# The first sort of a scan and two expert layers split in two, its first part beside the scan

## The reference

```
# attention: x, f_logit are (2, 5056, 256)
f = lower_bound + (1 - lower_bound) * sigmoid(f_logit);  i = 1 - f
for t in range(S):  h = f[:, t] * h + i[:, t] * x[:, t];  y[:, t] = h
# layer 0: N = 10112 tokens, D = 256, E = 8 experts, F = 1024
logits = (x/|x|) @ (emb/|emb|).T / tau;  expert_idx = argmax(logits)
out[mask_e] = gate_w * (relu(x[mask_e] @ w1[e]) @ w2[e])     # gate_w: softmax value of the chosen one
# layer 1: the same with logits = x @ w_gate and its own w1, w2
```

## Time and profile before

| | us |
|---|---|
| median of 3 runs | 1384.75 (1382.49 to 1385.55) |
| the profiled execution | 1383.36 |
| its span | 1381.6 |
| PE busy | 1329.6 (96%) |
| DVE busy | 971.5 (70%) |
| ACT busy | 835.2 (60%) |
| POOL busy | 439.2 (32%) |

### The profile page before, as it was taken

How to read it: one execution, slowest core, us unless ns; L and a number is a source line. 1 busy time by engine, 2 the same in 40 slices (tenths; PEclk the granted TensorE clock), 3 DMA queues, 4 the chain that set the end, 5 groups by cost and what they waited for, 6 DMA issues and landing times.

```text
span 1381.6 us, 31343 instructions
## 1 busy us (share of the span) xinstructions
PE 1329.6 (96%) x11005; PEld 1299.6 (94%) x11005; DVE 971.5 (70%) x1468; ACT 835.2 (60%) x1402; POOL 439.2 (32%) x458
## 2 busy tenths in 40 slices
PE   7994799999999999999999999999999999999996
PEld 6993399999999999999999999899999999999996
DVE  5878476666666666669876679777777777777773
ACT  4774166666666666666656566556666666666663
POOL 4663221121221211222111234323444444444431
PEclk9995599999999999999999999999999999999999
DMA  8983686666665656668856668546666666666650
GB/s 256 329 275 104 64 273 193 213 199 194 203 198 200 199 195 214 198 193 154 254 166 192 209 202 217 174 153 212 221 217 213 226 226 216 221 213 219 222 186 1
DMA packets 204662, 276.83 MB, mean 200 GB/s; under 512 B 33350, under 2 KB 171988, under 8 KB 204596
## 3 DMA queue, kind: packets, MB, share of 16 engines
q1 hardware_dynamic: 191060, 240.74, 56.7%
q0 software_dynamic: 13536, 35.21, 7.6%
HBM read 242.69 MB, written 35.18 MB: 201 GB/s over the span
## 4 chain that ended last, share of the span: by engine, by line
PE 91%; DVE 4%; issue 1%; ACT 1%; POOL 1%; DMA 1%; SPq 0%; ACTq 0%; DVEq 0%; POOLq 0%
PE bank L1306 39%; PE bank L1324 38%; PE bank L1240 4%; PE bank L1290 3%; PE bank L1335 2%; PE bank L1344 1%; PE bank L1203 1%; PE bank L1222 1%; PE bank L1216 1%; DVE hT L381 1%; DVE gx L371 1%; POOL fg L888 1%; ACT sq L1063 0%; DMA fin<-in_f_logit 0%; ACT th L1049 0%
## 5 line engine op out<-in xcount | busy, mean ns | idle before, releaser
L1306 PE MATMUL bank<-xs,w1h 128*128 128x256 f32 x3008 | 570.5, 288 | 1.5 <-DVE xs L656 1.5
L1119 ACT ACTIVATE hh<-bank 128x512 fp32r<-128x512 f32 x376 | 225.2, 599 | 413.6 <-PE bank L1306 413.6
L1306 PEld LDWEIGHTS bank<-xs,w1h 128*128 128x128 f32 x3008 | 461.5, 189 | 3.2 <-DVE xs L656 1.9
L667 DVE SCALAR_TENSOR_TENSOR hl<-bank,hh 128x512 fp32r<-128x512 f32 x376 | 259.9, 691 | 249.3 <-ACT hh L1119 246.9
L1324 PE MATMUL bank<-w2h,hl 128*128 128x256 f32 x1504 | 423.1, 281 | 0.0
L1324 PE MATMUL bank<-w2l,hh 128*128 128x256 f32 x1504 | 422.5, 281 | 0.0
L1324 PE MATMUL bank<-w2h,hh 128*128 128x256 f32 x1504 | 421.7, 280 | 0.0
L1306 PE MATMUL bank<-xs,w1l 128*128 128x256 f32 x1504 | 421.6, 280 | 0.0
L1306 PEld LDWEIGHTS bank<-xs,w1l 128*128 128x128 f32 x1504 | 283.7, 189 | 0.0
L1324 PEld LDWEIGHTS bank<-w2h,hh 128*128 128x128 f32 x1504 | 283.3, 188 | 0.0
L1324 PEld LDWEIGHTS bank<-w2l,hh 128*128 128x128 f32 x1504 | 283.1, 188 | 0.0
(11 more groups left out here) (160 smaller groups left out, 1039.6 us busy)
## 6 DMA issues: line engine op xcount, KB each, us to landing
w1raw<-in_moe_w SPq DMA_DIRECT2D x94, 1024.0 KB
w2raw<-in_moe_w SPq DMA_DIRECT2D x94, 1024.0 KB, 5.6
rows_b<-yb SPq DMA_DIRECT2D x94, 128.0 KB, 2.3
xin<-in_x SPq DMA_DIRECT2D x19, 512.0 KB, 6.0
fin<-in_f_logit SPq DMA_DIRECT2D x19, 512.0 KB, 7.9
rows_a<-h_rows SPq DMA_DIRECT2D x19, 512.0 KB, 5.6
xb<-rows_a,row_i POOLq DMA_INDIRECT x94, 4.9
xb<-rows_b,row_i POOLq DMA_INDIRECT x94, 4.9
```

The source lines that it names most:

```text
L667: v.scalar_tensor_tensor(hl[:, j, :], bank[j % UB][:, :], 0.0, hh[:, j, :].bitcast(fp32), ALU.max, ALU.subtract).then_inc(hid_lo, 1)
L1119: nc.scalar.activation(hh[:, j, :], bank[j % UB][:, :], ACT.Relu).then_inc(hid_hi, 1)
L1306: ins = mm(bank[j % UB][:, f * GW:(f + 1) * GW], w[:, p, o:o + P], xs[:, p, a, c * GW:(c + 1) * GW], start=k == 0, stop=k == 3 * DC - 1)
```

## The change

```diff
@@ scan, PE
                     for dst, src in ((bank[c], xin), (bank[2 + c], fin)):
+                        in_time = dst[:, 0:nt * P].rearrange("p (q j) -> p q j", j=nt)
                         for j in range(nt):
-                            ins = nc.tensor.transpose(dst[:, j * P:(j + 1) * P],
+                            ins = nc.tensor.transpose(in_time[:, :, j],
                                                       src[:, sx, j * D + c * P:j * D + (c + 1) * P],
                                                       ident[:, :])
@@ scan, PE (the other engines likewise)
             def a_step(i):
                 a_front(i, CH if i.var is not None else tiles_in(i.const))
+                tick(i)
+                tick(i)
                 if i.var is not None or i.const > 0:
                     a_back(i.plus(-1), CH)
-            run_steps(pe, 0, NCH, a_step, LOOP_K, 2)
+                tick(i)
...
+            def sort(q):
+                lo, hi, T, W = PARTS[q][0:4]
+                for _ in range(OH_AT[q] + 1):
+                    yield
+                for b, e, k, number in groups(q):
+                    if b == 0:
+                        pe.wait_ge(dve_c, mark["oh", q])
+                    else:
+                        pe.wait_ge(dve_c, mark["counted", q, b - 1])
+                    mm(sum_of(q, T), ones_b[:, :], oh[:, e:e + k, 0:T], start=True, stop=True)
+                    mm(cum_of(q, T), upto[:, :], oh[:, e:e + k, 0:T], start=True, stop=True).then_inc(pe_s, 1)
+                    yield
+                    yield
+                for _ in range(FRONT[q] + 1 - OH_AT[q] - 2 * len(groups(q))):
+                    yield
+                pe.wait_ge(dve_c, mark["counted", q, len(groups(q)) - 1])
+                for c, t0 in enumerate(range(0, T, RC)):
+                    g, w = c + CHUNK0[q], min(RC, T - t0)
+                    pe.wait_ge(lane_ok, g + 1)
+                    pe.wait_ge(valp_ok, g + 1)
+                    pe.wait_ge(valt_ok, g + 1)
+                    for t in range(w):
+                        ins = mm(table_of(q, T, W), lane_oh[:, g % RS, :, t], vals[:, g % RS, 0:2 * W, t],
+                                 start=t0 + t == 0, stop=t0 + t == T - 1)
+                    ins.then_inc(tab_ok, 1)
+                    yield
+                    if q >= 2 and c % 3 == 2:
+                        yield
+            parts = [sort(q) for q in range(2 * LY)]
+            tick = beside_scan(parts[0])
+            run_steps(pe, 0, K1 + 1, a_step, LOOP_K, 0)
+            for k in range(K1 + 1, NCH):
+                a_step(Index(k))
             a_back(Index(NCH - 1), tiles_in(NCH - 1))
-            routing()
-            pe.wait_ge(dve_c, mark["table read"])
-            tick = beside(resort(0), resort(1))
+            finish(parts[0])
+            tick = beside(parts)
+            pe.wait_ge(dve_c, mark["slots", 0])
@@ pairs, PE
-                if here(last2) and layer_of(last2) == 0:
-                    turn_y(last2, 1)
...
                 if here(i) and here(nxt):
                     turn_x(nxt)
+                if here(old) and layer_of(old) == 0:
+                    y_logits(old)
                 if here(last2) and layer_of(last2) == 0:
-                    y_logits(last2, 1)
+                    turn_y(last2)
@@ after the scan, DVE
+            for c in range(DC):
+                split_w1_lo(Index(0), c)
+            finish(parts[0])
+            for half in range(2):
+                split_w2_lo(Index(0), half)
+            tick = beside(parts)
             m_x(Index(0))
@@ scan and pairs, SP
+                if q == 0:
+                    sp.wait_ge(dve_c, mark["experts", q])
+                    for i in (Index(0), Index(1)):
+                        read_expert(i)
+                        load_w1(i)
+                        load_w2(i)
+                        yield
+                sp.wait_ge(dve_c, mark["pair", q])
+                sp.dma_start((rows_av if q < 2 else rows_bv)[:, lo:hi, D:D + 2], pair[:, lo:hi, :]
+                             ).then_inc(pair_out, 16)
...
+                if i.var is None and i.const == P1 - 3:
+                    sp.wait_ge(dve_c, mark["experts", 1])
@@ pairs, POOL
+                if i.var is None and i.const == P1 - 3:
+                    pool.wait_ge(dve_c, mark["slots", 1])
+                    pool.wait_ge(pair_out, 32)
```

More of the change, by code:

```diff
@@ L161, in build @@
+        fg = sb("fg", [P, DC, CW], fp32)
+        gx = sb("gx", [P, DC, CW], fp32)
+        sq = sb("sq", [P, 2, CH, D], bf16)
         RC = 8
         RS = 4
[L163 to L169, removed]
@@ L180, in build @@
[L180 to L186, removed]
+        WM = ST - G * min(P1, PA)
+        lane_oh = sb("lane_oh", [P, RS, P, RC], bf16)
+        tile_oh = sb("tile_oh", [P, RS, WM, RC], bf16)
+        vals = sb("vals", [P, RS, 2 * WM, RC], bf16)
@@ L1169, in step @@
                         split_w2_hi(nxt, 0)
-                if here(last) and layer_of(last) == 0:
-                    m_yT(last, 0)
-                tick(i, 2)
+                tick(i)
                 if here(i):
@@ L1227, in a_step @@
                 a_front(i, CH if i.var is not None else tiles_in(i.const))
+                tick(i)
+                tick(i)
                 if i.var is not None or i.const > 0:
                     a_back(i.plus(-1), CH)
-            run_steps(pe, 0, NCH, a_step, LOOP_K, 2)
-            a_back(Index(NCH - 1), tiles_in(NCH - 1))
-            def chunk(g, w, W, b, first, last):
-                pe.wait_ge(lane_ok, g + 1)
-                pe.wait_ge(valp_ok, g + 1)
-                pe.wait_ge(valt_ok, g + 1)
-                for t in range(w):
-                    ins = mm(bank[b][:, 0:2 * W], lane_oh[:, g % RS, :, t], vals[:, g % RS, 0:2 * W, t],
-                             start=first and t == 0, stop=last and t == w - 1)
-                ins.then_inc(tab_ok, 1)
@@ L1278, in resort @@
                     yield
-                    if q % 3 == 2:
+                    if q >= 2 and c % 3 == 2:
                         yield
+            parts = [sort(q) for q in range(2 * LY)]
+            tick = beside_scan(parts[0])
+            run_steps(pe, 0, K1 + 1, a_step, LOOP_K, 0)
+            for k in range(K1 + 1, NCH):
+                a_step(Index(k))
+            a_back(Index(NCH - 1), tiles_in(NCH - 1))
+            finish(parts[0])
+            tick = beside(parts)
             def turn_x(i):
@@ L1373, in step @@
                     down(i, 0)
-                if here(last) and layer_of(last) == 0:
-                    turn_y(last, 0)
-                tick(i, 2)
+                tick(i)
                 if here(i):
@@ L1379, in step @@
                     down(i, 1)
-                if here(last) and layer_of(last) == 0:
-                    y_logits(last, 0)
-                tick(i, 3)
+                tick(i)
             run_pairs(pe, step)
```

664 lines of the change are left out of this document (309 added, 355 removed).

## The result

| | before | after |
|---|---|---|
| median of 4 runs, us | 1384.97 (1382.49 to 1385.55) | 1408.48 (1406.88 to 1409.83) |
| profiled execution, its span | 1383.36, 1381.6 | 1409.83, 1408.1 |
| PE busy | 1329.6 (96%) | 1341.7 (95%) |
| DVE busy | 971.5 (70%) | 984.6 (70%) |

The ratio is 1.018, 95% interval 1.0164 to 1.0195. The forecast was 1382, its range 1371 to 1402.

The account below looks back on a forecast made before the run. PE was taken to bound both layers, with a serial stretch of 56.1 us after the scan. Terms -42.8 + 18.0 + 21.5 + 1.0 - 1.0 = -3.3 us gave 1381.5 against the median, forecast 1382 us, range 1371 to 1402.

Parts of the forecast that it names:

- step 3: Sort 1 beside pairs 0 to 8 of layer 0: 21.5 us more for PE, 1.0 us for its start in pair 0.
- step 2: Sort 0 (40 tiles) beside chunks 11 to 19 of the scan: makes the scan 18.0 us longer, bounds 14 and 25.
- step 4: Logits of layer 0 in one group a pair: -1.0 us over 47 pairs, bounds -5 and +3; last sorts 0.
- Step 1: Serial stretch between last logits and layer 0's first matmul shrinks from 56.1 to 13.3 us: -42.8 us.
- the bubble behind the second count: In the scan, PE's second count waits for DVE and holds up chunk 13's transposes: about 2.9 us within step 2.
- Rival A: Scan transposes writing every fourth PSUM column cost 0.234 us each: 26 us more, 1408 in all; chance 0.17.
- Rival C: PE's clock falls in the scan's second half: 22 us more, 1404, or 3 to 11 if it alternates; chance 0.10.
- B: Less taken back: no bubble or clock loss in the scan, cheaper pair 0 and merged logits: 9 us less, 1373; chance 0.15.
- D: Sort 0 not through by the scan's end: 3 to 6 us more, 1386; chance counted within the forecast's 0.58.
- the seam: The serial stretch from the scan's last logits to layer 0's first matmul, forecast to change by -42.8 us.

Follow-up runs that it names:

- e1: The changed kernel with SP's wait for the gate pairs of sorts 1 and 3 four ticks later; 1387.3 us, ratio 1.0016 against before.
- e4: e1 with sort 0 run whole after the scan, no tick of it beside the scan; 1384.58 us, ratio 1.0004 against before.
- e5: e4 with POOL's number tables made later and the first sort whole again (all 79 tiles, no sort 1); 1390.73 us, ratio 1.0047 against before.
- e11: e6 with sort 1 beside pairs 1 to 9 of layer 0 in place of 0 to 8; 1380.73 us, ratio 0.9985 against before.
- e8: e6 with an unused tensor of 32 bytes a partition ahead of some buffers, which shifts them; 1398.95 us in one run.
- e10: e6 with the ring of one-hot tables three entries deep in place of four, which moves buffers 5408 bytes lower; 1392.04 us in one run.
- e9: e6 with an unused tensor of 1024 bytes a partition ahead of the same buffers as in e8; 1384.25 us in one run.
- e3: e1 with PE turning h back twice in chunks 10 to 19 of the scan, same result; 1385.97 us, ratio 1.0028 against before.
- e7: e1 with POOL's number tables made later and PE's doubled transposes of e3; 1388.4 us, ratio 1.0024 against before.
- e12: The changed kernel, sort 0 beside the scan, with SP's wait later, number tables later and sort 1 a pair later; 1379.28 us, ratio 0.9967 against before.
- e6: e4 with POOL making its number tables only when DVE has scaled the embeddings; 1383.54 us, ratio 1.0 against before.

## Why the prediction was wrong

**The step that failed: step 3, in its clause on SP and POOL.** For sort 1 it priced PE's table, DVE's work and POOL's wait for the slots, and no word went to SP's wait for `mark["pair", q]`, though SP's piece of the generator is in the diff and every load of weights stands behind it. I had used the store of the gate pairs only to count SP's backlog in step 2. In step 4 I wrote that the last sorts keep their work and cost "0, and a wait of up to 3 us each if DVE is late": at sort 3 SP issued nothing for 24 us, which cost 11.4. Counting the pieces of both generators side by side would have given it: SP asks in call 12, DVE answers in call 16 of a sort with four groups. Price: 10.2 + 11.4 = 21.6 us (e1). None of the rivals had it. "PE shows idle time in the pairs" was named as what would show the forecast wrong, and that is what the trace shows.

**Step 1 holds.** 14.25 us from the last logits to the first up matmul, forecast 13.3. Rows of after, of all engines:

```profile
140.89 0.18 DVE L442 COPY logit<-bank 128x24 f32<-128x24 f32 x1 [4.37 <-PE bank L1209]
...
143.46 0.18 DVE L608 SCALAR_TENSOR_TENSOR slot_row<-small,bank 128x24 int32<-128x24 f32 x1
...
155.32 0.58 PE L1283 MATMUL bank<-xs,w1h 128*128 128x256 f32 x1 [1.41 <-DVE xs L626]
```

**Step 2 was mis-sized, 28.1 for 18.0 us, in its bubbles and at both ends of the scan.** Counted from e4, which has no sort beside the scan, DVE's share was right: 19.5 us busy and 2.0 in small gaps, forecast 21.2. The slack of 7.1 us was there too. e4's stretch is 2.6 us shorter than before's (by the new layout or by the chunks that now stand outside the loop, which was not separated), and its DVE still waits 4.6 us for fg, in eight short waits. With the sort beside it both are used up. But three long waits for fg stand in their place, 7.1 us in all, where the forecast had one bubble of 2.9. DVE's waits in that stretch of after and of e4, and the longest of them:

```profile
DVE gx L422 <- POOL fg L875: 7.1, 3, 3.4
```

```profile
DVE gx L421 <- POOL fg L874: 4.6, 8, 0.7
```

```profile
87.70 0.69 DVE L422 SCALAR_TENSOR_TENSOR gx<-fg,bank 128x512 f32<-128x512 f32 x1 [3.38 <-POOL fg L875]
```

This one is the bubble behind the second count, as foretold. The forecast had no wait at the first count, where PE stands 2.90 us for the one-hot. The granted clock falls during this wait and stays at half, so the transposes on which fg waits run slower (rows of PE, then the window with the clock in its third number from the end):

```profile
78.66 0.32 PE L1230 MATMUL bank<-oh,ones_b 128*128 128x160 bf16 x1 [2.90 <-DVE oh L495]
...
84.24 1.06 PE L1190 MATMUL bank<-ident,xin 128*128 128x128 f32 x4
```

```profile
77.40:87.60 10.20, 8.94 (x44) 8.88 (x45) 6.53 (x10) 3.14 (x11) 3.58 (x4) 0.50 0.62 199
```

The scan's end takes 2.1 us more than before, where the forecast had 1.0 for the clock in all. And the start lost 4.6 us in this execution. The number tables on POOL "fall in its idle time" and were priced at 0, but they held up an operation of DVE for which PE's first matmul waits, 2.1 us; the rest is the later rise of the clock, which is chance (e4 has the same tables and lost 0.1). In sum 21.5 - 7.2 + 7.1 + 2.1 + 4.6 = 28.1. The bound of 25 "if the slack can't be used at all" is near it for another reason.

**Step 3's table holds.** The chain has one group of eight matmuls of 140 columns at 2.06 us, 0.258 each, forecast 0.26:

```profile
262.58 2.06 PE bank L1243 x8
```

From pair 3 to 10 e1 has grown by 20.4 us. The start of sort 1 was priced at 1.0, bounds 0 to 4, and cost 4.3 (e5, e11).

**Step 4 was right by its own mechanism and missed another.** e5, e8 and e10 have the merged logits and gain 0.5 to 0.6 us over 39 pairs, 0.013 a pair; forecast 0.02. After gains 0.115 a pair there, and 0.09 in layer 1, where no logits are. That comes from where the buffers lie (e8, e9). I had not thought of it; it is some 7 us in favour of the change, by luck, and it hid part of the other losses.

**Rival A is refuted.** With every fourth column written, four transposes start 0.43 to 0.44 us apart, as in the earlier trace rows:

```profile
40.58 0.60 PE L1190 MATMUL bank<-ident,fin 128*128 128x128 f32 x4
41.01 0.60 PE L1190 MATMUL bank<-ident,xin 128*128 128x128 f32 x4
```

By the Trainium skill (Advanced Engine Details and Errata, PSUM Cachelines) this access should have cost; in this trace fp32 transposes that write with a stride of 16 bytes cost the same as contiguous ones, 0.11 us.

**Rival C** is true in its sign: the clock is 0.72 from chunk 11 to 19 (0.96 before), and 0.50 at the scan's end in e1. Its price of 22 us did not come: the whole step missed by 10, and e3 and e7 don't separate the clock's part.

**Rivals B and D** did not come. The bubble that B leaves out is there. For D sort 0 would not be through by the end of the scan; its slot row stands at 143.46, 2.4 us behind the last logits.

Together, measured less forecast: SP +21.6; step 2 +10.1, of it 4.6 at the start; the start of sort 1 +3.3; the seam +1.0; pairs 49 to 62 with sorts 2 and 3, not taken apart, +1.5; pair 3 to 10 -1.3; pair 10 to 49 -3.5; layer 1 -2.9. That is 29.8, from -3.3 to 26.5. e12, with three mends, comes out near the forecast (ratio 0.9967, 4.6 us less than before). That doesn't confirm the sum: the scan still takes some 28 us more in its profile, sort 1 runs a pair later, and the place of the buffers gives some 7.

## What to carry over

Where several engines walk through generators of pieces, count for each wait in which call it is asked and in which call it is answered, for every variant of the generator, and begin with the queue that only issues transfers: it looks idle and everything hangs on it. Slack read as the difference of a pace and an engine's busy time could be spent here, but the work put there made other engines wait for it, and it for them, in new and longer waits (7.1 us for a forecast of 2.9): ask for each piece who waits for it. This kernel, at the bound of one engine, has a spread of 0.1 us in a 13 us stage from the place of its buffers, some 7 us in all, as much as whole steps of the change: test an edit beside a version whose buffers lie the same.

## What was not expected of the hardware

- A shift of 32 bytes a partition of six buffers made a pair of layer 0 go from 12.96 to 13.07 us and one of layer 1 from 11.70 to 11.83; a shift of 1024 bytes changed neither.
- A DVE operation on 8 partitions and 256 elements took 2.65 us in place of 0.40 while POOL wrote two tables by IOTA, and ended 0.14 us after the second.
- A load of 1 MB of weights took 11.69 us from issue to landing when four of them and two stores went out within 8 us; the median of the w2raw loads over the whole kernel is 5.8.
- Executions of one program differ by up to 8 us (1379.2 to 1387.3 in e6). Part of it, by the profiles, is when PE's clock rises in the first 30 us. In the nine profiles that share the late tables, chunk 11's scan starts at 68.9 to 69.3 us where the first 48 transposes ran at half clock, and at 64.0 to 65.2 where 16 to 21 did.
